# Nine identity products, raw weights in place, a head in pairs, and an early branch in a fused attention and two-layer kernel

## The chip, the cores and the metric

One core of one Trainium2 chip runs the whole program. The metric is the device time of one execution in microseconds (us). The engines are PE (TensorE), PEld (TensorE's weight loads), DVE (VectorE), ACT (ScalarE), POOL (GpSimd) and SP (SyncE, which here issues every DMA). Each engine works through its own instructions in the order written; semaphores order them between engines.

## The reference

Three stages. Attention is a gated recurrence over 768 steps for each of 4 x 8 heads with 48 dimensions; its output is the input of two feed-forward layers of 384 -> 2048 -> 384 over 3072 tokens.

```python
f = 1 / (1 + exp(-f_logit))
for t in range(S):                                  # attention
    state = f[t, :, None] * state + outer(k[t], v[t])
    y[t] = q[t] @ state
h = x @ w_in                                        # layer 1, g is a quadratic spline of h
g = where(h >= 1, h, where(h <= -1, 0, (h + 1)**2 / 4)); x = g @ w_out
h = x @ w2_in                                       # layer 2, g is a rational function of h
g = (a0 + a1*h + a2*h**2 + a3*h**3) / (1 + |b0|*|h| + |b1|*h**2 + 1e-6); out = g @ w2_out
```

## The kernel before

**Attention** is computed in chunks of 128 steps. An *item* is one chunk of one group of 8 heads (4 batches x 2 heads): 6 chunks x 4 groups = 24 items; `chunk_of(i)` names them. For an item ACT turns the gate logits into decay steps (`gate_steps`, L586), DVE multiplies them up (`scan`, L826), ACT and DVE form the inverse (`invert` L599, `newton` L845, `scale_queries` L859), POOL scales the keys (`scale_keys`, L497). PE computes scores (L1031), DVE masks them (L868), PE computes `outputs` (L1047) and transposed keys (`transposes`, L1018), ACT copies these (`copy_keys`, L611), PE forms `deltas` (L1067) and DVE adds them to the `states` (L879). ACT's `round_y` (L619) and DVE's `rest_y` (L893) split y into two fp32r parts, x_hi and x_lo. Part of y is moved between partitions by twelve small DMAs (`move_fourth`, L378).

**The layers** take blocks of 512 tokens, 6 blocks. Every product is three fp32r products: w_hi x_hi, w_hi x_lo and w_lo x_hi. Layer 1 has 16 *tiles* of 128 hidden rows per block, n = 0 to 95: `spline_first(n)` and `spline_second(n)` are nine matmuls of 512 columns each, and ACT and DVE compute the spline between them (`spline_in`, `spline_join`, `spline_hi`, `spline_lo`). Items 4 to 23 are worked into the loop over n, one per window of four tiles: `window_of(n)` gives item 4 + n // 4 and a stage 0 to 3. Stage 0 has the item's transposes and scores, stage 2 its outputs and deltas, stage 3 its rest_y and states. `transposes(i)` for i > 4 wait until item i - 1's states are done. Layer 2 has 8 *units* of 256 hidden rows per block (`rational_first`, `rational_second`, 18 matmuls each, the second four units after the first), and ACT, DVE and POOL steps per unit (`rational_step`).

**Weights** come in 16 pieces per layer (0 to 7 of the first matrix, 8 to 15 of the second; 384 KB each). SP loads a piece into one of two raw buffers, ACT copies it to w_hi rounded (`split_w1`, `split_w2`), POOL subtracts the rest into w_lo in three parts. `ORDER1`, `ORDER2` and `STEPS2` are the orders and steps by hand. Layer 2's pieces take the places of layer 1's: ten are split during layer 1's last block (at steps t in `STEPS2`), six in units 0 to 5 of layer 2's first block. The next block's x is split by ACT and POOL in units 4, 5 and 6 (`split_x2`).

**The head** is what comes ahead of the loop over n: items 0 to 3 and the start of item 4, each engine's order written out (PE from L1181, ACT from L756, DVE from L956, POOL from L560, SP from L408). **The end**: every engine reads a flag that DVE has set in layer 1's last block (growth in range) and jumps over a general program if all is well.

The functions that the change touches, and what calls them:

Of the kernel before, what the change touches and what calls it, by code (L numbers as in the profile page):

```python
# [58 lines left out]
ORDER1 = [m + UNITS * out for m in range(UNITS) for out in range(2)]  # L59
# [9 lines left out]
X2_STEPS = [3, 4, 6]  # L69

# [37 lines left out]
def build(nc, qT, kT, fT, vT, fC, kC, qC, vC, w1, w2, a, b, outT):  # L108
# [3 lines left out]
    with ctx:  # L112
# [9 lines left out]
        w_lo = lay.tile("w_lo", PIECES * WPC, F32R)  # L122
        x_hi = lay.tile("x_hi", [P, KT, 2 * NB], F32R)
# [3 lines left out]
        w_raw = [lay.tile(f"w_raw{u}", WPC) for u in range(2)]  # L127
# [105 lines left out]
        w1_loaded = [sem(f"w1_loaded{r}") for r in range(2)]  # L233
        w1_hi_done = sem("w1_hi_done")
        w1_lo_done = sem("w1_lo_done")
        w2_loaded = [sem(f"w2_loaded{r}") for r in range(2)]
# [94 lines left out]
        def _(sp):  # L331
# [32 lines left out]
            def load_w1(k):  # L364
                if k >= 2:
                    sp.wait_ge(w1_lo_done, SPLITS * (k - 1))
                at = ORDER1[k] * WPC
                sp.dma_start(w_raw[k % 2][:, :], w1[:, at:at + WPC]).then_inc(w1_loaded[k % 2], 16)

            def load_w2(k):  # L370
                if k >= 2:
                    sp.wait_ge(w2_lo_done, SPLITS * (k - 1))
                else:
                    sp.wait_ge(w1_lo_done, SPLITS * PIECES)
                at = ORDER2[k] * WPC
                sp.dma_start(w_raw[k % 2][:, :], w2[:, at:at + WPC]).then_inc(w2_loaded[k % 2], 16)
# [54 lines left out]
            load_f(5)  # L431
            move_fourth(0)
# [4 lines left out]
            load_w1(2)  # L437
            load_q(5)
            load_w1(3)
            load_v(5)  # L440
            load_w1(4)
            sp.dma_start(a_bc[:, :], a.rearrange("(o a) -> o a", o=1).to_broadcast([P, 4])).then_inc(coef_loaded, 16)
            sp.dma_start(b_bc[:, :], b.rearrange("(o a) -> o a", o=1).to_broadcast([P, 2])).then_inc(coef_loaded, 16)
            for n in range(N1):
# [10 lines left out]
                if n + HEAD_PIECES + 2 < PIECES:  # L455
                    load_w1(n + HEAD_PIECES + 2)
                if n % TILES == LAG1 + 1 and n >= TILES:
                    store1(n // TILES - 1)
                t = n - (N1 - TILES)
                if t == 0:  # L460
                    load_x2(0)
                if t in (0, 1):
                    load_w2(t)
                if t in STEPS2:
                    load_w2(STEPS2.index(t) + 2)
            load_x2(1)
            for k in range(len(STEPS2) + 2, PIECES):
                load_w2(k)
# [5 lines left out]
            store2(BLOCKS - 1)  # L474
            sp.wait_ge(flag_set, 1)
            flag = sp.value_load(okflag[0:1, 0:1], min_val=0, max_val=P)
            sp.wait_ge(stored2, 16 * KT * BLOCKS)
            with sp.If(flag < P):
                general.sync_program(sp, qT, kT, fT, vT, xT, x1T, w1, w2, outT)

        @block.gpsimd
        def _(pool):
# [26 lines left out]
            def split_w1(k):  # L509
                pool.wait_ge(w1_hi_done, k + 1)  # L510
                for part in range(SPLITS):
                    own = slice(part * WPC // SPLITS, (part + 1) * WPC // SPLITS)
                    at = slice(ORDER1[k] * WPC + own.start, ORDER1[k] * WPC + own.stop)
                    nc.gpsimd.tensor_tensor(w_lo[:, at], w_raw[k % 2][:, own], w_hi[:, at].bitcast(F32),
                                            ALU.subtract).then_inc(w1_lo_done, 1)

            def split_w2(k):
                m = ORDER2[k]
                pool.wait_ge(w2_hi_done, k + 1)
                if m < UNITS:  # L520
                    pool.wait_ge(h1_ready, N1 - TILES + UW * (m + 1))
                else:
                    pool.wait_ge(multiplied1, N1 - TILES + UW * (m - UNITS + 1))
                for part in range(SPLITS):
                    own = slice(part * WPC // SPLITS, (part + 1) * WPC // SPLITS)
                    at = slice(m * WPC + own.start, m * WPC + own.stop)
                    nc.gpsimd.tensor_tensor(w_lo[:, at], w_raw[k % 2][:, own], w_hi[:, at].bitcast(F32),  # L527
# [37 lines left out]
            split_w1(1)  # L565
            scale_keys(4)
            split_w1(2)
            for n in range(N1):
                i, stage = window_of(n)
                if n + HEAD_PIECES < PIECES:  # L570
                    split_w1(n + HEAD_PIECES)
# [445 lines left out]
        def _(pe):  # L1017
# [179 lines left out]
            for n in range(N1):  # L1197
                i, stage = window_of(n)
                spline_first(n)
                if n == 0:  # L1200
                    deltas(3)
# [298 lines left out]
```

## Time and profile before

| | us |
|---|---|
| median of 3 runs | 930.59 (928.19 to 931.43) |
| the profiled execution | 931.32 |
| its span, first to last instruction | 929.6 |
| PE busy | 894.3 (96%) |
| PEld / DVE / ACT / POOL busy | 737.5 / 666.1 / 632.3 / 277.8 |
| mean granted PE clock | 0.985 of full |

The rows of the profile give a start, a duration, the engine, the source line, and what is written from what, with the number of instructions; the brackets at the end hold the idle time of the engine ahead of the instruction and what ended it. Durations of matmuls overlap: the time from one start to the next is what a matmul costs. An fp32 matmul is recorded as two. A busy PE is not a PE at its peak.

### The profile page before, as it was taken

Reading aid. Unit: us, or ns where it says so; the run is one execution under the profiler, and the core shown is the slowest. Engines: PE = TensorE matmul, PEld = TensorE weight load, DVE = VectorE, ACT = ScalarE, POOL = GpSimd, SP = SyncE. Lnnn points to the kernel's source line nnn. Section 1 sums busy time; section 2 is a strip of 40 time slices with the busy share of each in tenths; the row PEclk is TensorE's granted clock in tenths of the full one; section 3 lists DMA queues with packets and bytes.
Section 4 is the critical chain, followed back from the end, with each engine's and each line's share of the span. In section 5 each row is a group of like instructions: output and inputs, shape, how many; then the busy total and the mean of one; then the engine's idle time right before and its main releaser. Section 6 shows DMA issues by size and latency. Waiting matters only on the chain.

```text
span 929.6 us, 13243 instructions
## 1 busy us (share of the span) xinstructions
PE 894.3 (96%) x4786; PEld 737.5 (79%) x4786; DVE 666.1 (72%) x813; ACT 632.3 (68%) x821; POOL 277.8 (30%) x202
## 2 busy tenths in 40 slices
PE   4799999999999999999999998999999999999996
PEld 3577788888888888888888886888888888888884
DVE  7866656655655566565344799889899889889883
ACT  5566665556555655655577796888787888887881
POOL 3455500000010000000055487235344244353223
PEclk9699999999999999999999998999999999999999
DMA  6434313212211211110233221001001001000001
GB/s 190 117 96 133 103 35 97 58 35 62 59 35 36 85 55 49 58 37 1 69 102 88 83 68 35 1 35 34 0 34 34 23 11 34 34 0 0 34 0 38
DMA packets 27513, 48.72 MB, mean 52 GB/s; under 512 B 5312, under 2 KB 8384, under 8 KB 27456
## 3 DMA queue, kind: packets, MB, share of 16 engines
q1 hardware_dynamic: 27456, 48.00, 17.3%
q8 instruction: 31, 0.51, 0.2%
q14 instruction: 26, 0.21, 0.1%
HBM read 36.18 MB, written 9.44 MB: 49 GB/s over the span
## 4 chain that ended last, share of the span: by engine, by line
PE 79%; DVE 8%; ACT 5%; issue 4%; POOL 3%; POOLq 0%; DMA 0%; SPq 0%; DVEq 0%; ACTq 0%
PE acc L1121 18%; PE acc L1165 18%; PE h_pair L1104 17%; PE at_pair L1143 10%; PE h_pair L1143 10%; PE at_pair L1044 2%; DVE growth L838 2%; PE at_pair L1063 2%; PE at_pair L1058 2%; DVE g L909 1%; POOL g_lo L548 1%; POOL w_lo L527 1%; ACT t L656 1%; ACT t L653 1%; DVE guess L856 1%
## 5 line engine op out<-in xcount | busy, mean ns | idle before, releaser
L548 POOL TENSOR_TENSOR g_lo<-g,g_hi 128x1024 fp32r<-128x1024 f32 x48 | 116.7, 2432 | 222.9 <-DVE t L938 218.4
L909 DVE SCALAR_TENSOR_TENSOR g<-h_pair,t 128x512 f32<-128x512 f32 x96 | 66.4, 691 | 142.1 <-ACT t L656 141.9
L653 ACT ACTIVATE t<-h_pair,half 128x512 f32<-128x512 f32 x96 | 66.0, 688 | 101.1 <-PE h_pair L1104 99.9
L1104 PE MATMUL h_pair<-x_hi,w_hi 128*128 128x512 f32 x288 | 113.6, 394 | 2.8 <-DVE x_lo L902 2.5
L507 POOL TENSOR_TENSOR k_s<-k_in,growth 128x512 f32<-128x512 f32 x22 | 29.0, 1316 | 289.0 <-DVE growth L838 288.2
L1165 PE MATMUL acc<-g_hi,w_hi 128*128 128x512 f32 x288 | 112.5, 390 | 1.9 <-POOL g_lo L548 1.9
L1104 PE MATMUL h_pair<-x_hi,w_lo 128*128 128x512 f32 x288 | 112.9, 392 | 0.0
L1104 PE MATMUL h_pair<-x_lo,w_hi 128*128 128x512 f32 x288 | 112.8, 392 | 0.0
L1165 PE MATMUL acc<-g_lo,w_hi 128*128 128x512 f32 x288 | 112.1, 389 | 0.0
L1165 PE MATMUL acc<-g_hi,w_lo 128*128 128x512 f32 x288 | 112.1, 389 | 0.0
L1121 PE MATMUL acc<-g_hi,w_hi 128*128 128x512 f32 x264 | 107.5, 407 | 0.0
L663 ACT CAST g_hi<-g 128x512 fp32r<-128x512 f32 x88 | 54.6, 621 | 75.3 <-DVE g L909 75.2
L1121 PE MATMUL acc<-g_hi,w_lo 128*128 128x512 f32 x264 | 103.2, 391 | 0.0
L1121 PE MATMUL acc<-g_lo,w_hi 128*128 128x512 f32 x264 | 102.9, 390 | 0.0
L917 DVE TENSOR_TENSOR g_lo<-g,g_hi 128x512 fp32r<-128x512 f32 x88 | 63.0, 716 | 46.7 <-ACT g_hi L663 46.7
L929 DVE SCALAR_TENSOR_TENSOR s<-s,b_abs,g 128x1024 f32<-128x1024 f32 x48 | 66.6, 1388 | 37.8 <-ACT g L709 37.7
L527 POOL TENSOR_TENSOR w_lo<-w_raw,w_hi 128x256 fp32r<-128x256 f32 x48 | 48.1, 1030 | 69.9 <-ACT w_hi L647 66.3
L1104 PEld LDWEIGHTS h_pair<-x_hi,w_hi 128*128 128x128 f32 x288 | 54.5, 189 | 15.4 <-DVE x_lo L902 3.0
L953 DVE SCALAR_TENSOR_TENSOR g<-g,a_bc,t 128x1024 f32<-128x1024 f32 x48 | 65.5, 1364 | 0.0
L1165 PEld LDWEIGHTS acc<-g_hi,w_hi 128*128 128x128 f32 x288 | 54.1, 188 | 14.2 <-POOL g_lo L548 3.1
L1104 PEld LDWEIGHTS h_pair<-x_hi,w_lo 128*128 128x128 f32 x288 | 54.5, 189 | 11.5
L1104 PEld LDWEIGHTS h_pair<-x_lo,w_hi 128*128 128x128 f32 x288 | 54.5, 189 | 11.2
(142 smaller groups left out, 2053.9 us busy)
## 6 DMA issues: line engine op xcount, KB each, us to landing
w_raw<-w SPq DMA_DIRECT2D x32, 384.0 KB, 3.4
f_in<-fC SPq DMA_DIRECT2D x48, 96.0 KB, 2.9
k_in<-kC SPq DMA_DIRECT2D x48, 96.0 KB, 2.4
q_in<-qC SPq DMA_DIRECT2D x48, 96.0 KB, 2.3
mlp_out<-o_sb SPq DMA_DIRECT2D x18, 256.0 KB, 3.3
x_raw<-mlp_out SPq DMA_DIRECT2D x6, 768.0 KB, 4.4
outT<-o_sb SPq DMA_DIRECT2D x18, 256.0 KB, 2.0
v_in<-vC SPq DMA_DIRECT2D x22, 192.0 KB, 2.5
```

What stands on the lines that cost most here:

```text
L527: nc.gpsimd.tensor_tensor(w_lo[:, at], w_raw[k % 2][:, own], w_hi[:, at].bitcast(F32), ALU.subtract).then_inc(w2_lo_done, 1)
L548: nc.gpsimd.tensor_tensor(g2_lo[r][:, :, :], g2[r][:, :, :], g2_hi[r][:, :, :].bitcast(F32), ALU.subtract).then_inc(lo2_ready, 1)
L653: nc.scalar.activation(t1[n % 2][:, :], h1[n % 2], ACT.Relu, scale=0.5, bias=half[:, :]).then_inc(relu1_ready, 1)
L663: nc.scalar.copy(hi, g1[n % 2][:, :]).then_inc(hi1_ready, 1)
L909: nc.vector.scalar_tensor_tensor(out=g1[n % 2][:, :], in0=h1[n % 2], scalar=1.0, in1=t1[n % 2][:, :], op0=ALU.max, op1=ALU.min).then_inc(g ...
L917: nc.vector.tensor_tensor(lo, g1[n % 2][:, :], hi.bitcast(F32), ALU.subtract).then_inc(lo1_ready, 1)
L929: nc.vector.scalar_tensor_tensor(out=s, in0=s, scalar=b_abs[:, 1:2], in1=g, op0=ALU.mult, op1=ALU.add).then_inc(den_ready, 1)
L953: nc.vector.scalar_tensor_tensor(out=g_before, in0=g_before, scalar=a_bc[:, 0:1], in1=t_before, op0=ALU.add, op1=ALU.mult).then_inc(g2_rea ...
L1104: mm = nc.tensor.matmul(h1[n % 2], w[:, at:at + P], x[:, kt, cols], start=(kt == 0 and j == 0), stop=(kt == KT - 1 and j == 2))
L1121: mm = nc.tensor.matmul(acc[o][:, :], w[:, at:at + P], g, start=(t == 0 and j == 0), stop=(t == TILES - 1 and j == 2))
L1143: mm = nc.tensor.matmul(h2[m % 2][:, c * NB:(c + 1) * NB], w[:, at:at + P], x[:, kt, xcols], start=(k == 0), stop=(k == 3 * KT - 1))
L1165: mm = nc.tensor.matmul(acc[o][:, :], w[:, at:at + P], g[m % R2][:, c, :], start=(m == 0 and c == 0 and k == 0), stop=(last and c == UW - ...
```

## The change

It has six parts. (1) `keep_busy`: six fp32 products of the identity with itself ahead of item 2's scores and three ahead of item 3's, into the scores' own PSUM bank, read by nobody and overwritten by the scores. (2) The raw weights lie in w_lo's memory, each piece at its own place with its own semaphore; a load of layer 1 waits for nothing, a load of layer 2 until the old piece has been used. Layer 1's pieces alternate between the matrices. (3) The head is written in pairs: items 2 and 3 together, and the first four tiles and item 4 of the loop unrolled and reordered on ACT, DVE and PE. (4) In the loop, layer 1's pieces are split one tile later. (5) Layer 2's last six pieces go to units 0, 1, 2, 3, 7 and 8 instead of 0 to 5. (6) SP reads the flag ahead of its last store and jumps ahead of the wait for that store; ACT reads it ahead of layer 2.

```diff
-ORDER1 = [m + UNITS * out for m in range(UNITS) for out in range(2)]
+ORDER1 = [0, 1, 8, 2, 9, 3, 10, 4, 11, 5, 12, 6, 13, 7, 14, 15]
+LATE_PIECES = {0: [10], 1: [11], 2: [12], 3: [13], 7: [14], 8: [15]}
         w_lo = lay.tile("w_lo", PIECES * WPC, F32R)
+        lay.at -= 4 * PIECES * WPC
+        w_raw = lay.tile("w_raw", PIECES * WPC)
...
-        w_raw = [lay.tile(f"w_raw{u}", WPC) for u in range(2)]
...
             def load_w1(k):
-                if k >= 2:
-                    sp.wait_ge(w1_lo_done, SPLITS * (k - 1))
-                at = ORDER1[k] * WPC
-                sp.dma_start(w_raw[k % 2][:, :], w1[:, at:at + WPC]).then_inc(w1_loaded[k % 2], 16)
+                at = slice(ORDER1[k] * WPC, (ORDER1[k] + 1) * WPC)
+                sp.dma_start(w_raw[:, at], w1[:, at]).then_inc(w1_loaded[k], 16)
             def load_w2(k):
-                if k >= 2:
-                    sp.wait_ge(w2_lo_done, SPLITS * (k - 1))
+                m = ORDER2[k]
+                if m < UNITS:
+                    sp.wait_ge(h1_ready, LAST_BLOCK + UW * (m + 1))
                 else:
-                    sp.wait_ge(w1_lo_done, SPLITS * PIECES)
+                    sp.wait_ge(multiplied1, LAST_BLOCK + UW * (m - UNITS + 1))
...
+            load_w1(2)
             move_fourth(0)
...
-                if t in (0, 1):
-                    load_w2(t)
-                if t in STEPS2:
-                    load_w2(STEPS2.index(t) + 2)
+                if t + 1 in STEPS2:
+                    load_w2(STEPS2.index(t + 1))
...
-            store2(BLOCKS - 1)
             sp.wait_ge(flag_set, 1)
             flag = sp.value_load(okflag[0:1, 0:1], min_val=0, max_val=P)
+            store2(BLOCKS - 1)
+            with sp.If(flag < P):
+                sp.wait_ge(stored2, 16 * KT * BLOCKS)
+                general.sync_program(sp, qT, kT, fT, vT, xT, x1T, w1, w2, outT)
             sp.wait_ge(stored2, 16 * KT * BLOCKS)
-            with sp.If(flag < P):
-                general.sync_program(sp, qT, kT, fT, vT, xT, x1T, w1, w2, outT)
...  # POOL's and ACT's split_w2 no longer wait for h1_ready or multiplied1
-            late_pieces = range(len(STEPS2), PIECES)
-            for off, piece in enumerate(late_pieces):
-                rational_step(0, off, [piece])
+            for off in range(UNITS + 1):
+                rational_step(0, off, LATE_PIECES.get(off, ()))
...  # ACT, from round_y(0)
-            copy_keys(0) round_y(1) split_w1(0) invert(3) copy_keys(1) round_y(2) copy_keys(2)
-            gate_steps(4) split_w1(1) round_y(3) invert(4) copy_keys(3) split_w1(2) gate_steps(5)
-            for n in range(N1 + LAG1):
+            copy_keys(0) invert(3) round_y(1) copy_keys(1) gate_steps(4) split_w1(0) split_w1(1)
+            round_y(2) round_y(3) copy_keys(2) copy_keys(3) split_w1(2) gate_steps(5)
+            spline_in(0) invert(4) spline_hi(0) spline_in(1) spline_hi(1) copy_keys(4) split_w1(3)
+            spline_in(2) spline_hi(2) invert(5) split_w1(4) spline_in(3) spline_hi(3) round_y(4)
+            gate_steps(6) split_w1(5)
+            for n in range(WINDOW, N1 + LAG1):
...
+            act.wait_ge(flag_set, 1)
             flag = act.value_load(okflag[0:1, 0:1], min_val=0, max_val=P)   # now ahead of layer 2
...  # DVE, from mask(1)
-            rest_y(0) newton(2) scale_queries(2) scan(3) rest_y(1) mask(2) newton(3)
-            scale_queries(3) rest_y(2) mask(3) scan(4) rest_y(3) states(0) newton(4)
-            scale_queries(4) states(1) states(2) states(3)
+            scan(3) rest_y(0) newton(2) scale_queries(2) newton(3) scale_queries(3) mask(2) mask(3)
+            rest_y(1) rest_y(2) rest_y(3) states(0) states(1) scan(4) states(2) states(3)
+            spline_join(0) newton(4) spline_lo(0) scale_queries(4) spline_join(1) mask(4)
+            spline_lo(1) scan(5) spline_join(2) spline_lo(2) newton(5) scale_queries(5)
+            spline_join(3) rest_y(4) states(4) spline_lo(3)
...  # PE
+            def keep_busy(i, count):
+                for _ in range(count):
+                    nc.tensor.matmul(scores_at(i)[0][0][:, 0:P], ident[:, :], ident[:, :], start=True, stop=True)
...  # PE, from transposes(1)
-            scores(2) deltas(0) outputs(2) transposes(2) scores(3) deltas(1) outputs(3)
-            transposes(3) deltas(2)
+            deltas(0) keep_busy(2, 6) scores(2) keep_busy(3, 3) scores(3) outputs(2) outputs(3)
+            transposes(2) transposes(3) deltas(1) deltas(2)
+            spline_first(0) deltas(3) spline_first(1) transposes(4) spline_first(2)
+            spline_second(0) scores(4) spline_first(3) second_half(4) spline_second(1)
```

## Rows read from the trace of the kernel before

**Rows 1.** The page's first part: busy us, share of the span, instructions.
```profile
PE 894.3 (96%) x4786; PEld 737.5 (79%) x4786; DVE 666.1 (72%) x813; ACT 632.3 (68%) x821; POOL 277.8 (30%) x202
```

**Rows 2.** TensorE by stretch: length, busy, granted clock, DMA share, GB/s.
```profile
24.10:26.40 2.30, 0.00 (x0) 1.00 0.18 39
27.00:27.50 0.50, 0.50 (x10) 0.77 0.23 45
...
44.00:44.50 0.50, 0.50 (x5) 0.66 0.46 129
...
574.10:580.00 5.90, 5.90 (x14) 0.50 0.46 133
```

**Rows 3.** The timeline of TensorE in the head.
```profile
38.42 0.79 PE L1104 MATMUL h_pair<-x_hi,w_hi 128*128 128x512 f32 x1 [1.90 <-DVE x_lo L902]
...
49.72 1.05 PE L1058 MATMUL at_pair<-q_s,state 128*128 128x128 f32 x8
50.70 1.08 PE L1063 MATMUL at_pair<-probs,v_in 128*48 128x128 f32 x16
...
58.36 0.39 PE L1104 MATMUL h_pair<-x_hi,w_hi 128*128 128x512 f32 x1
...
62.12 0.63 PE L1028 MATMUL at_bank<-ident,k_s 128*128 128x128 f32 x4 [1.56 <-DVE state L891]
```

**Rows 4.** The chain of waits: start, length, what.
```profile
124.98 2.34 PE h_pair L1104 x9
...
131.13 2.04 PE h_pair L1104 x9
...
642.53 4.08 PE at_pair L1143 x18
```

**Rows 5.** The timeline of TensorE and GpSimd around layer 2's start.
```profile
474.23 2.13 POOL L527 TENSOR_TENSOR w_lo<-w_raw,w_hi 128x256 fp32r<-128x256 f32 x3 [3.53 <-PE h_pair L1104]
...
549.74 2.41 POOL L548 TENSOR_TENSOR g_lo<-g,g_hi 128x1024 fp32r<-128x1024 f32 x1 [1.25 <-DVE t L938]
552.11 5.09 POOL L527 TENSOR_TENSOR w_lo<-w_raw,w_hi 128x256 fp32r<-128x256 f32 x3
...
574.05 0.79 PE L1143 MATMUL at_pair<-x_hi,w_hi 128*128 x1 [3.22 <-POOL x_lo L537]
...
581.15 0.39 PE L1165 MATMUL acc<-g_hi,w_hi 128*128 128x512 f32 x1
...
638.83 2.35 POOL L537 TENSOR_TENSOR x_lo<-x_raw,x_hi 128x512 f32 x1
```

**Rows 6.** The end: last stores, then single instructions by line (ns, start us).
```profile
920.69 3.05 SPq L406 DMA_DIRECT2D outT<-o_sb  x3
...
L478 SPq COMPARE_BRANCH  x1: 50/50/50, 926.6 to 926.6; - x1
...
L112 ACTq DRAIN  x1: 80/80/80, 926.8 to 926.8; - x1
L112 SPq DRAIN  x1: 48/48/48, 929.3 to 929.3; - x1
...
L810 ACTq TENSOR_LOAD <-okflag x1: 743/743/743, 922.8 to 922.8; - x1
```

**Rows 7.** The timeline of VectorE in the head.
```profile
22.20 1.36 DVE L838 TENSOR_TENSOR_SCAN growth<-growth,zero 128x128 f32<-128x128 f32 x4
...
33.94 2.58 DVE L838 TENSOR_TENSOR_SCAN growth<-growth,ends,zero 128x128 f32<-128x128 f32 x4 [1.27 <-ACT growth L597]
...
36.97 1.40 DVE L902 TENSOR_TENSOR x_lo<-at_bank,x_hi 48x512 fp32r<-48x512 f32 x2
```

**Rows 8.** ScalarE in layer 1's last block; layer 2's loads from issue to landing.
```profile
481.50 0.68 ACT L653 ACTIVATE t<-h_pair,half 128x512 f32<-128x512 f32 x1
...
486.77 0.83 ACT L647 CAST w_hi<-w_raw 128x768 fp32r<-128x768 f32 x1
...
DMA to landing us min/median/max: 2.9/3.3/5.4
```

More of the change, by code:

```diff
@@ L511, in split_w1 @@
                 for part in range(SPLITS):
-                    own = slice(part * WPC // SPLITS, (part + 1) * WPC // SPLITS)
-                    at = slice(ORDER1[k] * WPC + own.start, ORDER1[k] * WPC + own.stop)
-                    nc.gpsimd.tensor_tensor(w_lo[:, at], w_raw[k % 2][:, own], w_hi[:, at].bitcast(F32),
+                    at = slice(ORDER1[k] * WPC + part * WPC // SPLITS, ORDER1[k] * WPC + (part + 1) * WPC // SPLITS)
+                    nc.gpsimd.tensor_tensor(w_lo[:, at], w_raw[:, at], w_hi[:, at].bitcast(F32),
                                             ALU.subtract).then_inc(w1_lo_done, 1)
@@ L964, in _ @@
             mask(1)
+            scan(3)
             rest_y(0)
@@ L967, in _ @@
             scale_queries(2)
[L968 to L970 removed]
             newton(3)
             scale_queries(3)
+            mask(2)
+            mask(3)
+            rest_y(1)
             rest_y(2)
[L974 to L975 removed]
             rest_y(3)
             states(0)
[L978 to L979 removed]
             states(1)
+            scan(4)
             states(2)
             states(3)
[L983 removed]
+            spline_join(0)
+            newton(4)
+            spline_lo(0)
+            scale_queries(4)
+            spline_join(1)
+            mask(4)
+            spline_lo(1)
+            scan(5)
+            spline_join(2)
+            spline_lo(2)
+            newton(5)
+            scale_queries(5)
+            spline_join(3)
+            rest_y(4)
+            states(4)
+            spline_lo(3)
+            for n in range(WINDOW, N1):
                 i, stage = window_of(n)
@@ L1186, in _ @@
             transposes(1)
+            deltas(0)
+            keep_busy(2, 6)
             scores(2)
-            deltas(0)
+            keep_busy(3, 3)
+            scores(3)
             outputs(2)
+            outputs(3)
             transposes(2)
-            scores(3)
+            transposes(3)
             deltas(1)
-            outputs(3)
-            transposes(3)
             deltas(2)
-            due = 0
-            for n in range(N1):
+            spline_first(0)
+            deltas(3)
+            spline_first(1)
+            transposes(4)
+            spline_first(2)
+            spline_second(0)
+            scores(4)
+            spline_first(3)
+            second_half(4)
+            spline_second(1)
+            due = LAG1
+            for n in range(WINDOW, N1):
                 i, stage = window_of(n)
                 spline_first(n)
-                if n == 0:
-                    deltas(3)
                 if stage == 0:
@@ L1205, in _ @@
                     second_half(i)
-                if n >= LAG1 and n not in HOLD:
+                if n not in HOLD:
                     spline_second(due)
```

97 lines of the change are left out of this document (47 added, 50 removed).

## The prediction

> **What bounds the kernel now.** I read the shares first, then the granted clock by stretch, then each engine's instructions at the three places where TensorE is not busy. [rows 1] give TensorE 894.3 of 929.6 us busy, so only its gaps and its low clock can be won. [rows 2] show the two low stretches. TensorE did nothing from 24.10 to 26.40; the granted clock then fell at 27.0 to 27.5 from 1.00 to 0.50, which is 1.2 instead of 2.4 GHz, and came back at 44.0 to 44.5. It also worked at 0.50 from 574.1 to 580, behind a second gap. [rows 3] follow the head: first product of spline tile 0 at 38.42, released by VectorE; tile 4 at 58.36; the transposes of item 5 at 62.12 after 1.56 us of waiting for the state sums. From 124.98 (tile 16) on, groups of nine products follow each other every 2.04 us and the rational units of four such groups every 8.16 [rows 4]: there TensorE is the bound. The second gap is the wait of 3.22 us in [rows 5] for GpSimd's x_lo, because GpSimd had 5.09 us of weight split, 2.35 of x_lo and 2.41 of g_lo, 9.85 in a unit of 8.16. The third loss is the end in [rows 6]: a branch at 926.6, the drain at 929.3.
>
> **The head.** Added: nine fp32 identity products. The nearest row of that shape (128x128 weights, 128 columns) is the state product in [rows 3]: 8 records, two per product, in 0.98 us from its start to its follower's at 50.70, so 0.245 us each, 1.47 for six and 0.74 for three. Other bound: they cost nothing where TensorE waits anyway. The rest is order. I walk the new one with durations of [rows 3, 7] and of the same groups of the head at the full clock.
>
> Until 18.9 us nothing changes. VectorE then does scan 3 (1.36), the rest of y 0 (0.61), and two items' inverses and queries (2.05 each): queries 2 are ready at 23.0, queries 3 at 25.1. TensorE has item 1's transposes done at 21.8, item 0's deltas (0.47) at 22.3, six products until 23.8, scores 2 (1.09) until 24.9, three products until 25.6, scores 3 until 26.7. Masks 2 and 3 (1.20 each) end at 26.3 and 27.95, outputs 2 at 27.8 and 3 at 29.1, transposes at 30.2. Three times 1.42 for the rests of y 1 to 3 end at 32.2; the moved rows of x, issued as before, are there by then. So spline tile 0 starts at 32.3, 6.1 earlier, and at the full clock: TensorE's longest gap since 19.9 is under 1 us, where the old one was 2.4. The nine products lie in the wait for the queries except 0.6 us, which VectorE's masks inherit and which is in the walk.
>
> Then tile 0 until 34.3, deltas 3, tile 1 until 36.8. Scan 4 (up to 2.58 beside GpSimd) ends at 36.0, its keys (1.28) at 37.3, transposes 4 at 37.9, tile 2 at 40.4, second product 0 at 42.4, scores 4 at 43.5, tile 3, outputs and deltas 4 (2.36) at 47.9, second product 1 at 50.0, tile 4 at 52.1. The old tile 4 ended at 60.4. This is 8.3 us ahead, but the vector side isn't: mask 4 must wait for scores 4 (43.6 to 44.8), then come lo 1, scan 5 (until 47.4), join 2 (48.0), ScalarE's hi 2, inverse 5 (1.29), weight split (0.74) and tile 3 (1.3) until 52.0, join 3, hi 3, rounding of y 4 (0.50), rest of y 4 and state sums 4 until 56.3. TensorE's transposes of item 5 wait for these sums: from 52.1 to 56.3, 4.2 us instead of 1.56. Queued behind this wait are scores 5 and all spline products; ScalarE and VectorE wait for them. **Gain at this point: 62.12 - 56.3 = 5.8 us.** Carried on with the same durations to tile 16, it is 6.8 (118.2 against 124.98), since the next two waits for state sums shrink to 0 and 0.7. The same arithmetic in the old order gives tile 4 at 58.1 and tile 16 at 124.7, where the rows have 58.36 and 124.98. With no slowing of VectorE beside GpSimd it gives a gain of 5.2; the bounds are 5.2 and 6.8, and I take 6.8, as the rows do show that slowing (scan 2.58 against 1.36).
>
> This holds if the clock stays up. Gaps of 2.4 and 3.2 us were each followed by 0.50 [rows 2], so I expect it to fall in this 4.2 us gap, and to come back some 6 us after work resumes, as it did after 574.05. At half rate transposes, scores and a spline group take 1.04 + 1.7 + 3.84 instead of 0.56 + 1.09 + 2.04, 2.9 us; if a second group is caught, 4.7. Of the 6.8 remain 3.9 or 2.1. **I take 3.5.**
>
> By the Trainium skill, TensorE: Matmul & The Clock Gate (Part 1, the section on what is actually happening), the number of matmuls before the clock is released varies between runs of one kernel. The trace agrees as far as one execution can: 7.0, 5.7 and 6.1 us of work preceded the three rises. By that rule the 3.9 and the 2.1 can both occur in runs of the same kernel.
>
> **The first weights.** Raw pieces now land in w_lo's own place, so no load waits for a split, and the pieces' order alternates. ScalarE casts 13 pieces in the windows as before (three of them in the unrolled part), one tile later each; each first-matrix piece is ready three tiles before its use, each second-matrix piece about two. What hides this is that distance. Taken 0; bounds 0 and +0.8 (one cast of 0.83, as in [rows 8], on the path once).
>
> **The second weights in place.** The load of a piece now waits until the old piece is no longer read, and two raw buffers no longer run ahead. The tightest is piece 3: tile 87's product is there at 481.50 at the latest, the cast starts at 486.77, 5.3 us later; loads land in 3.3 us, at most 5.4 [rows 8]. Taken 0; bounds 0 and 0.2 us for each of seven such pieces, 1.4. SP's queue behind these waits holds only the next pieces, load_x2 and the last stores, none of them due within 8 us. ScalarE's earlier read of the flag costs 0.74 + 0.17 + 0.02 (the first of them in [rows 6]) at 509.9, where it delays unit 0; TensorE uses the result four units later (32 us), so 0.
>
> **The late pieces.** Pieces 14 and 15 move from units 4 and 5 to units 7 and 8. GpSimd in units 4 to 6 then has 2.41 + 2.35 = 4.8 us, as in every later block, and in 7 and 8 2.41 + 5.09 = 7.5, both under 8.16. In a later block the third x_lo ends at 641.2, 1.3 us ahead of its matmul at 642.5 [rows 4, 5]. Here pieces 12 and 13 have already put item 2's g_lo 1.4 us late (549.74), and VectorE, the cause, has 0.7 us idle per later unit to win it back: the third x_lo ends between 569.8 and 570.8, its matmul is due at 570.67. So the gap goes but for 0.2 at most, too short for the clock: the group behind it starts at 570.67 + 4.08 = 574.75 instead of 581.15 [rows 5]. **Gain 6.4 us**: 3.4 of gap with its restart, 3.0 of low clock. Next late would be the second products of units 6 and 7, which need pieces 14 and 15 at 591 and 599; the splits end near 572 and 580. Lower bound 3.2, if a shorter wait stays.
>
> By the Trainium skill, GPSIMD Engine Reference (1, Specifications), GpSimd's SBUF interface is shared with VectorE and contended by vector instructions with two SBUF inputs. This speaks against putting the pieces into units 7 and 8, where VectorE is 90% busy. The trace agrees: three splits took 5.09 there and 2.13 elsewhere [rows 5]. Taken at 2.13, units 4 and 5 would never have been late; at 5.09 the new place still fits.
>
> **The end.** SP's flag read moves ahead of the last store and the branch ahead of the wait for it. Before: last issue done at 923.74, wait for landing until 926.6, branch, 2.6 us to the drain [rows 6]. After: branch at 923.8, 2.6 us, landing at 926.6 meanwhile, end near 926.9 instead of 929.6. ScalarE's branch comes 1.0 earlier (drain near 925.9). Gain 2.6; the jump may be slower beside the store's traffic, down to 1.5. **I take 2.5.**
>
> **Sum.** 3.5 + 6.4 + 2.5 = 12.4. The profiled execution took 931.32, 1.7 more than its span; it stands 0.7 above the median 930.59 and inside 928.19 to 931.43. 931.32 - 12.4 = 918.9; half of the 0.7 off for the median: **918.5 us**.
>
> **Rivals.**
> 1. The clock survives the gap at 52 us. For: TensorE is dense on both sides; against: both old gaps, which were shorter. Head 6.8, sum 15.7, 915.6 us.
> 2. The nine products don't hold the clock at 27 us. For: they are small, and some waits stay around them; against: TensorE is over 85% busy from 19.9 on. Then the clock is low from 27 to 44 as before; the same walk puts tile 16 at 125.3, 0.5 later than the old order: sum 8.4, 922.9 us.
> 3. The gap at 571 stays, since the third x_lo has only 1.3 us of slack in the steady state and starts here 1.4 late. For: these two numbers; against: what units 4 and 5 no longer do. Sum 6.0, 925.3 us; a gap of 1 us without a fall of the clock leaves 5.4 of the 6.4.
> 4. Slower: layer 2's loads. Once they can't start before the old piece is free, ScalarE, which casts between two tiles, stops for each of seven pieces, and TensorE with it. Slack is 1.9 us over the usual 3.3; it decides from 5.3, and costs all of the 12.4 at 7.1 us per load (seven times 1.8). At 7.8 us per load, 918.5 + 7 x 2.5 = 936 us. Against: the longest of 16 was 5.4.
>
> **How the numbers follow.** Forecast 0.55, rival 1 0.20, rival 2 0.12, rival 3 0.06, rival 4 0.03, something unseen 0.04. Range: the forecast's own is 916.5 to 921; I reach to rival 1 with all terms at their best, 913.5, and past rival 2 to 924.5. A measurement of this kernel tells about 0.3%, 2.8 us, from no change. Faster takes the forecast, rivals 1, 2 and nearly all of 3: 0.93; the same 0.04; slower 0.03.
>
> **What would show it.** Head: granted clock 1.00 from 27 to 44, tile 0 near 32.3, transposes 5 near 56.3 after a wait of about 4 us, 0.50 behind it, tile 16 near 121. Transition: no gap and no 0.50 between 505 and the last unit, the third x_lo of block 1 done before 570.7. End: last landing to the drain under 0.5 us. Wrong would be: 0.50 at 27 to 44; ScalarE waiting for w_raw loads; a wait for x_lo at unit 8; a start of tile 16 later than 124.98.

## The result, and the profile after

| | us |
|---|---|
| changed kernel, median of 4 runs | 919.29 (918.73 to 920.17) |
| kernel before, median of 4 runs | 930.88 (928.19 to 931.43) |
| ratio | 0.9882 [0.9860, 0.9904] |
| profiled execution / its span | 920.17 / 918.4 |

The kernel became 1.2% faster, 11.6 us by the medians. The numbers in brackets behind a ratio are its 95% interval. The changed kernel's four runs form two pairs: 918.73 twice, at a mean granted clock of 0.997, and 919.84 and 920.17 at 0.995; the profiled one is the slowest. The two profiled spans, 929.6 and 918.4, differ by 11.2: 3.0 us in the head, 5.6 at layer 2's start, 2.6 at the end. The forecast of 918.5 had 3.5, 6.4 and 2.5, 12.4 in all.

The page of the changed kernel, first part, against [rows 1]:

```profile
PE 890.6 (97%) x4804; PEld 734.9 (80%) x4804; DVE 663.7 (72%) x813; ACT 632.3 (69%) x821; POOL 276.9 (30%) x202
```

TensorE has 18 more records (nine fp32 products of two each) and is nevertheless busy for 3.7 us less, since less of its work runs at the low clock. The windows on TensorE, against [rows 2] (length, busy, granted clock, DMA share, GB/s):

```profile
27.00:44.00 17.00, 15.16 (x144) 1.00 0.61 176
...
53.00:57.00 4.00, 0.53 (x4) 0.96 0.17 62
57.00:64.00 7.00, 7.00 (x31) 0.53 0.23 52
...
115.00:123.00 8.00, 6.05 (x27) 1.00 0.33 93
...
560.00:582.00 22.00, 21.45 (x95) 1.00 0.12 36
```

The stretch from 27 to 44, which was at 0.50, is at 1.00. One low stretch is left in the head, behind the gap at 53; the one in layer 2 has gone. The timeline of TensorE, against [rows 3]:

```profile
21.61 1.60 PE L1103 MATMUL acc<-ident 128*128 128x128 f32 x12
23.76 1.16 PE L1066 MATMUL acc<-q_s,o_sb 48*128 48x128 f32 x16 [0.54 <-DVE q_s L873]
24.85 0.94 PE L1103 MATMUL at_bank<-ident 128*128 128x128 f32 x6
...
32.62 0.50 PE L1131 MATMUL h_pair<-x_hi,w_hi 128*128 128x512 f32 x1 [0.34 <-DVE x_lo L910]
...
56.56 0.78 PE L1050 MATMUL at_bank<-ident,k_s 128*128 128x128 f32 x3 [3.47 <-DVE state L899]
```

Spline tile 0 starts at 32.62 instead of 38.42; item 5's transposes at 56.56 instead of 62.12. Tile 16, in the chain of waits against [rows 4], starts at 121.95 instead of 124.98. The chain gives what released it:

```profile
118.44 0.69 DVE q_s L862
...
119.15 0.70 DVE guess L864
...
120.49 0.68 DVE x_lo L910
...
121.20 0.70 DVE x_lo L910
...
121.95 2.34 PE h_pair L1131 x9
```

VectorE sets this point, with the next item's query steps (q_s, guess) ahead of the x_lo that tile 16 needs; TensorE waits 1.95 us for it. At layer 2's start the timelines of GpSimd, VectorE and TensorE, against [rows 5], read:

```profile
549.04 2.29 POOL L535 TENSOR_TENSOR x_lo<-x_raw,x_hi 128x512 fp32r<-128x512 f32 x1
...
565.67 2.27 POOL L535 TENSOR_TENSOR x_lo<-x_raw,x_hi 128x512 fp32r<-128x512 f32 x1
...
573.96 5.09 POOL L525 TENSOR_TENSOR w_lo<-w_raw,w_hi 128x256 fp32r<-128x256 f32 x3
...
550.10 2.31 DVE L937 SCALAR_TENSOR_TENSOR s<-s,b_abs,g 128x1024 f32<-128x1024 f32 x1
...
592.40 1.28 DVE L937 SCALAR_TENSOR_TENSOR s<-s,b_abs,g 128x1024 f32<-128x1024 f32 x1
...
568.34 0.49 PE L1170 MATMUL at_pair<-x_hi,w_hi 128*128 x1 [0.55 <-POOL x_lo L535]
```

The wait for x_lo is 0.55 us where it was 3.22. The end in the timeline, against [rows 6]:

```profile
912.07 3.05 SPq L409 DMA_DIRECT2D outT<-o_sb  x3
...
913.74 0.39 PE L1192 MATMUL acc<-g_hi,w_lo 128*128 128x512 f32 x1
914.16 0.60 ACT L682 ACTIVATE o_sb<-acc 128x512 f32<-128x512 f32 x1 [0.76 <-PE acc L1192]
```

And the branch, among the single instructions by line (ns, start us):

```profile
L479 SPq COMPARE_BRANCH  x1: 50/50/50, 915.2 to 915.2; - x1
```

SyncE now branches at 915.2, as soon as its last store is issued (912.07 + 3.05), and no longer waits for it to land first. From the end of TensorE's last product to the end of the span it is 918.4 - 914.13 = 4.3 us; before it was 6.8 (929.6 - 922.75).

### The profile page after: what moved, and what is told of

The parts are those of the page before. It is cut to its first block, busy times and chain, and to the rows that moved or that the text cites. A ratio compares the mean times of both kernels' runs of the same rounds, so it can differ in the third digit from the quotient of the medians.

```text
span 918.4 us, 13245 instructions
## 1 busy us (share of the span) xinstructions
PE 890.6 (97%) x4804; PEld 734.9 (80%) x4804; DVE 663.7 (72%) x813; ACT 632.3 (69%) x821; POOL 276.9 (30%) x202
## 4 chain that ended last, share of the span: by engine, by line
PE 81%; DVE 9%; ACT 4%; issue 4%; POOL 1%; POOLq 0%; DMA 0%; DVEq 0%; SPq 0%; ACTq 0%
PE acc L1148 19%; PE acc L1192 18%; PE h_pair L1131 17%; PE at_pair L1170 10%; PE h_pair L1170 10%; PE at_pair L1066 2%; PE at_pair L1085 2%; DVE growth L846 2%; PE at_pair L1080 2%; DVE g L917 1%; POOL g_lo L546 1%; ACT t L649 1%; ACT t L646 1%; PE at_bank L1050 1%; DVE probs L885 1%
## 5 line engine op out<-in xcount | busy, mean ns | idle before, releaser
L937 DVE SCALAR_TENSOR_TENSOR s<-s,b_abs,g 128x1024 f32<-128x1024 f32 x48 | 69.4, 1446 | 31.8 <-ACT g L702 31.7
L961 DVE SCALAR_TENSOR_TENSOR g<-g,a_bc,t 128x1024 f32<-128x1024 f32 x48 | 63.6, 1326 | 0.0
L1192 PEld LDWEIGHTS acc<-g_hi,w_lo 128*128 128x128 f32 x288 | 54.0, 188 | 11.2
```

The costliest lines, as they stand in the source:

```text
L937: nc.vector.scalar_tensor_tensor(out=s, in0=s, scalar=b_abs[:, 1:2], in1=g, op0=ALU.mult, op1=ALU.add).then_inc(den_ready, 1)
L961: nc.vector.scalar_tensor_tensor(out=g_before, in0=g_before, scalar=a_bc[:, 0:1], in1=t_before, op0=ALU.add, op1=ALU.mult).then_inc(g2_rea ...
L1192: mm = nc.tensor.matmul(acc[o][:, :], w[:, at:at + P], g[m % R2][:, c, :], start=(m == 0 and c == 0 and k == 0), stop=(last and c == UW - ...
```

## The experiments

Each was timed in turn with the kernel before on the same chip, and the ratios compare the two; medians of different chips are not compared directly. "By ratio" below means the ratio, or the difference of two ratios, times 930 us.

| run | median us (runs) | before us | ratio |
|---|---|---|---|
| e1_no_products | 920.57 (4) | 929.89 | 0.9891 [0.9874, 0.9907] |
| e2_products_old_order | 930.01 (12) | 929.89 | 0.9997 [0.9982, 1.0013] |
| e3_fill_gap | 918.83 (4) | 929.89 | 0.9877 [0.9862, 0.9892] |
| e4_sums_early | 918.40 (4) | 929.89 | 0.9874 [0.9859, 0.9889] |
| e5_late_alone | 924.88 (5) | 931.30 | 0.9929 [0.9915, 0.9943] |
| e7_pieces_earlier | 917.98 (4) | 931.30 | 0.9871 [0.9853, 0.9889] |
| e9_fill_both | 917.19 (4) | 931.30 | 0.9853 [0.9838, 0.9868] |
| e10_sums_fill_pieces | 915.98 (5) | 931.30 | 0.9839 [0.9826, 0.9853] |
| e6_end_alone | 927.72 (12) | 929.31 | 0.9981 [0.9969, 0.9993] |
| e11_in_place_alone | 930.06 (12) | 929.31 | 1.0013 [1.0001, 1.0025] |
| e12_best_no_products | 916.45 (4) | 929.31 | 0.9862 [0.9847, 0.9876] |
| e13_head_only | 925.22 (8) | 929.95 | 0.9957 [0.9942, 0.9972] |

**What are the nine products worth?** Two runs: the changed kernel without them, and the kernel before with them.

```diff
-            keep_busy(2, 6)
-            keep_busy(3, 3)      # e1; e2 adds both ahead of scores(2) and scores(3) in the old order
```

> The changed kernel without its nine identity products; all else is kept. Theory A (the products hold TensorE's clock in the head): the granted clock falls to 0.50 somewhere between 24 and 30 us and comes back near 44; tile 0 and what follows run at half rate until then, tile 16 starts near 125 instead of 121.95, and the time is 923 to 924 us. Rival B (the order in pairs alone is dense enough, the products only fill a wait): the clock stays at 1.00, tile 16 starts within 0.5 of 121.95, the time is 919 us.

> The kernel before with the nine identity products at the same two places (six ahead of item 2's scores, three ahead of item 3's); order, weights and the rest as before. Theory A (products and order are both needed): the gap behind item 0's deltas is only cut from 2.4 to some 1.5 us, the clock falls near 27 as before, and the time stays at 930 to 932 us. Rival B (products alone hold the clock): 1.00 at 30 us, tile 4 starts near 53.5 instead of 58.36, but the vector side gives most of it back in a longer wait at item 5's transposes (3.6 us, and a fall of the clock there): 928 to 930 us.

The windows on TensorE without the products (e1):

```profile
26.00:27.00 1.00, 1.00 (x18) 0.96 0.19 37
27.00:30.00 3.00, 3.00 (x31) 0.50 0.24 54
30.00:32.00 2.00, 2.00 (x30) 0.92 0.58 173
```

The clock does fall without them, at 26.9 where it fell at 27.3 before, but it is back after 3.4 us and not after 17. Tile 16 starts at 122.95 instead of 121.95: 1.0 us. By the ratios the products are worth 0.8 us, and that difference alone is not told apart from nothing. Theory A's fall came, its 923 to 924 us didn't. In the old order (e2):

```profile
27.00:30.00 3.00, 3.00 (x20) 0.50 0.24 53
30.00:32.00 2.00, 1.96 (x34) 0.93 0.63 185
...
36.00:40.00 4.00, 1.70 (x4) 0.64 0.53 151
40.00:44.00 4.00, 4.00 (x26) 0.51 0.16 28
```

Here the low stretch of 17 us is two shorter ones, the second behind the wait of 3.2 us for x_lo ahead of tile 0, and the time is unchanged (tile 16 at 124.83; before 124.98). The products need not have done that: e6 below has the old head without them, and its profile too has two stretches (10.2 and 3.4 us). TensorE is at 1.00 from 30.3 to 37.1 in e2, and tile 0 still starts at 38.30 (before 38.42), released by VectorE's x_lo: up to tile 0 the old head waited for VectorE, and its low clock there was hidden. So it is the order that brings tile 0 from 38.4 to 33.3 us in e1 and ends the stretch from 27 to 44; the products take at most a short stretch away.

**What does the gap at 53 us cost?** e3 fills it with thirteen more such products; e4 shortens it, by putting item 4's rounding and state sums ahead of item 5's inverse on ScalarE and VectorE.

```diff
+                if n == WINDOW:
+                    fill(13)                # e3: ident x ident into at_pair, ahead of transposes(5)
...
-            newton(5) scale_queries(5) spline_join(3) rest_y(4) states(4) spline_lo(3)    # e4, DVE
+            rest_y(4) states(4) newton(5) scale_queries(5) spline_join(3) spline_lo(3)
-            invert(5) split_w1(4) spline_in(3) spline_hi(3) round_y(4)                    # e4, ACT
+            round_y(4) invert(5) spline_in(3) split_w1(4) spline_hi(3)
```

> The changed kernel with 13 more unread identity products (0.248 us each, 3.2 us) in the 3.47 us in which TensorE waits for item 4's state sums ahead of item 5's transposes. Nothing is made ready earlier. Theory A (what this gap costs is the clock behind it): granted clock 1.00 from 56 to 64 us, tile 16 near 118.5 instead of 121.95, time 915.5 to 916.5 us. Rival B (the cost is the wait itself, since ScalarE and VectorE set the pace here): clock at 1.00, but tile 16 within 1 us of 121.95 and the time above 918 us.

> The changed kernel with the wait itself taken away: VectorE does the rest of y and the state sums of item 4 ahead of item 5's inverse, ScalarE rounds y of item 4 ahead of its inverse 5, and the weight split follows tile 3's first step. Theory A (the wait costs nothing, only the clock behind it; ScalarE and VectorE then set the pace up to tile 16): transposes 5 start at 53.1 with no wait, the clock stays at 1.00, later waits of 1 to 2 us come at items 6 and 7, tile 16 near 118, time 915.5 to 916.5 us, the same as when the gap is filled. Rival B (the wait is worth its 3.5 us too): tile 16 near 115, time 912 to 913 us.

The filled kernel (e3) in the timeline of TensorE:

```profile
52.96 3.06 PE L1108 MATMUL at_pair<-ident 128*128 128x128 f32 x26
56.63 0.63 PE L1050 MATMUL at_bank<-ident,k_s 128*128 128x128 f32 x4 [0.61 <-DVE state L899]
```

in its windows:

```profile
57.00:64.00 7.00, 7.00 (x44) 1.00 0.23 52
...
119.00:122.50 3.50, 3.50 (x9) 0.51 0.08 25
```

and in its chain of waits:

```profile
118.85 3.91 PE h_pair L1136 x9
```

The chain of the reordered one (e4):

```profile
118.46 2.35 PE h_pair L1131 x9
```

and its window:

```profile
119.00:122.50 3.50, 3.50 (x29) 1.00 0.00 1
```

The transposes start no earlier in e3 (56.63), only the clock is kept, and tile 16 comes 3.1 us earlier, at 118.85. In these two profiles that is the whole of the 2.9 us that I had put on the low clock. e4, which shortens the waits for state sums from 3.6 to 2.1 us in all and keeps the clock, gets tile 16 to 118.46, only 0.4 earlier than e3: VectorE sets the pace up to there. But neither run is 3 us faster than the changed kernel; by ratio they gain 0.5 to 0.7, and the 915.5 to 916.5 us of both theories A were missed. Two things account for that. The first is in the changed kernel itself: the profile of e7, a kernel with the same head (its edit is in layer 2), has the low stretch behind the same gap, but of 3.4 us, where the changed kernel's lasted 6.8:

```profile
57.00:64.00 7.00, 7.00 (x37) 0.76 0.24 53
...
120.31 0.50 PE L1131 MATMUL h_pair<-x_hi,w_hi 128*128 128x512 f32 x1 [2.00 <-DVE x_lo L910]
```

Its tile 16 starts at 120.31, so keeping the clock here is worth 1.5 us in some executions and 3.1 in others; the changed kernel's two pairs of runs, 1.1 to 1.4 us apart, would fit that, though only one of the four has a trace. The second: in e3's profile the 2.0 us of waiting ahead of tile 16 was followed by 0.50, and its nine products took 3.91 us instead of 2.34. In e4's profile (916.67 us) the same gap was followed by 1.00; its three other runs took 918.2 to 918.6 at a lower mean clock (0.997 to 0.998 against 0.999), which would fit the fall, but they left no trace. By the Trainium skill, TensorE: Matmul & The Clock Gate (Part 1, the section on what is actually happening), the point of release varies between runs of one kernel. The trace agrees: behind one gap of one head the clock came back after 3.4 us in e7's profile and after 6.8 in the changed kernel's. The fall varies here too: the gap ahead of tile 16 lost the clock in e3's profile and kept it in e4's.

**Both gaps filled.** e9 is e3 with seven products more, ahead of tile 16.

```diff
+                if n == TILES:
+                    fill(7)
```

> The changed kernel with fp32 identity products written as the others: thirteen ahead of item 5's transposes (the gap at 53 us) and seven ahead of tile 16's first product (the 2.0 us gap at 117 us that was followed by clock 0.50 when only the first gap was filled). Theory A (each low stretch behind a gap costs about half its length; the gap itself costs nothing because VectorE sets the pace): granted clock 1.00 from 20 us to beyond tile 16, tile 16's group 2.0 to 2.4 us long, time 916.9 (918.83 less 1.9), in all 2.3 to 2.8 under the changed kernel's 919.3. Theory B (the products push the work behind them and what the clock gives is taken back by VectorE or GpSimd later): 918.5 to 919.3, with tile 16's group at 2.3 and a longer wait elsewhere before 130 us. Seven products cost 1.7 us where the gap is shorter than that, so up to 0.3 later if the gap is 1.5.

The timeline of TensorE:

```profile
116.65 1.72 PE L1108 MATMUL at_pair<-ident 128*128 128x128 f32 x14
118.81 0.50 PE L1136 MATMUL h_pair<-x_hi,w_hi 128*128 128x512 f32 x1 [0.43 <-DVE x_lo L910]
```

and the window around it:

```profile
115.00:123.00 8.00, 7.57 (x53) 1.00 0.18 49
```

Theory A holds: tile 16 at 118.81, clock 1.000 in all four runs, which lie within 0.4 us of each other. By ratio it is 2.2 us faster than e3, and 2.7 faster than the changed kernel.

**The transition.** e5 moves the late pieces in the kernel before and nothing else. e7 moves pieces 11, 12 and 13 of the changed kernel one unit earlier.

```diff
-            late_pieces = range(len(STEPS2), PIECES)                                     # e5
+LATE_PIECES = {0: [10], 1: [11], 2: [12], 3: [13], 7: [14], 8: [15]}
...
-LATE_PIECES = {0: [10], 1: [11], 2: [12], 3: [13], 7: [14], 8: [15]}                     # e7
+LATE_PIECES = {0: [10, 11], 1: [12], 2: [13], 7: [14], 8: [15]}
```

> The kernel before with nothing changed but the units of layer 2's last six pieces: 0, 1, 2, 3, 7 and 8 instead of 0 to 5. Theory A (the gap at 571 us comes from pieces 14 and 15 in units 4 and 5, and the change took 5.6 us there): 5.6 less than before, 924.3 against 929.9, and no stretch at granted clock 0.50 in layer 2; with all 6.4 us of my step, 923.5. Rival (part of the gap went because raw weights lie in place and GpSimd no longer waits for the old piece's products): 3 to 4.5 less, 925.5 to 927, and a wait over 1 us for x_lo at unit 8.

> The changed kernel with layer 2's late pieces 10 and 11 both in unit 0, 12 in unit 1, 13 in unit 2, 14 and 15 in units 7 and 8 as in it. Theory A (the 0.6 us wait for x_lo at unit 8 is GpSimd's lag behind, brought on by piece 13 in unit 3, and VectorE has no time left to win it back): the wait is 0.1 or less and the time 0.6 to 0.8 under the changed kernel's, 918.5 to 918.7. Theory B (GpSimd starts each g_lo when VectorE has t ready, so its place comes from VectorE's own pace and not from the pieces): the wait stays at 0.5 to 0.6, 919.2 to 919.4. Bad case: two pieces in unit 0 make TensorE wait there for second products 0 by 1 to 3 us.

The first product of unit 8, which waits for x_lo, in the timeline of e5:

```profile
571.24 0.49 PE L1142 MATMUL at_pair<-x_hi,w_hi 128*128 x1 [0.54 <-POOL x_lo L538]
```

and of e7, where no wait is left:

```profile
566.01 0.39 PE L1170 MATMUL at_pair<-x_hi,w_hi 128*128 x1
```

e5 gained 6.6 us [5.3, 7.9] by ratio (6.4 by medians), and has the wait of 0.54 of the changed kernel: the rival that laid part of this on the raw weights falls, since they aren't in place here. e7's profile has no wait and tells theory A right; its time is 1.0 us below the changed kernel by ratio, and that alone is inside the interval. Its profiled 917.71 us can't be set against the changed kernel's 920.17 for these pieces, since 1.6 us of that is the shorter low stretch in the head shown above.

**The end alone** (e6), and **the raw weights alone** (e11).

```diff
-            store2(BLOCKS - 1)                                                           # e6, SP
             sp.wait_ge(flag_set, 1)
             flag = sp.value_load(okflag[0:1, 0:1], min_val=0, max_val=P)
-            sp.wait_ge(stored2, 16 * KT * BLOCKS)
+            store2(BLOCKS - 1)
             with sp.If(flag < P):
+                sp.wait_ge(stored2, 16 * KT * BLOCKS)
...
+        lay.at -= 4 * PIECES * WPC                                                       # e11
+        w_raw = lay.tile("w_raw", PIECES * WPC)
-                if k >= 2:
-                    sp.wait_ge(w1_lo_done, SPLITS * (k - 1))
```

> The kernel before with SyncE's flag read ahead of its last store and its branch ahead of the wait for that store, and ScalarE's flag read ahead of layer 2. Theory A (SyncE's taken branch of 2.6 us goes beside the landing of the store): last TensorE product to the end of the span 4.2 to 4.3 us instead of 6.84, time 2.5 less than before. Rival (the branch becomes slower beside the store's traffic, or ScalarE's own branch ends last): 1 to 1.9 less, with ScalarE's drain as the last record.

> The kernel before with its raw weights in w_lo's place and nothing else of the change: a load of layer 1 waits for nothing, one of layer 2 for the last product of the old piece, and neither ScalarE nor GpSimd waits for those products again. Theory A (my step: nothing): within 0.8 us of before. Rival 1 (my slower case: ScalarE stands for the loads that now start later): 1.4 to 17 more, with waits of ScalarE for w_raw in layer 1's last block. Rival 2 (it helps: loads in the head start earlier and the first splits with them): 1 to 2 less.

In e6's profile the last product ends at 919.63 and the span at 923.9: 4.3 us, as theory A has it. Its median came out 1.8 us below before by ratio, [0.7, 2.9], which doesn't contradict 2.6 but doesn't show it either. The reason why twelve runs don't settle 2.6 us is in the same profile, at layer 2's start, first in the timeline:

```profile
573.61 0.49 PE L1146 MATMUL at_pair<-x_hi,w_hi 128*128 x1 [3.21 <-POOL x_lo L539]
```

then in the window behind it:

```profile
574.00:580.00 6.00, 6.00 (x28) 1.00 0.42 131
```

The gap of 3.2 us is there, and the clock stays at 1.00 behind it, where [rows 2] have 0.50 for 5.9 us. So the 3.0 us of low clock in this place are paid in some executions and not in others (in e11's and e13's profiles the stretch there is 3.4 us long instead of 6.8), and runs of the kernel before lie between 926.4 and 932.1 at mean clocks of 0.994 to 0.983. e11 is 1.2 us slower than before by ratio, [0.1, 2.3]. Its waits are those of before: TensorE's tile 16 at 124.93, 3.2 us for x_lo, no wait of ScalarE for w_raw in layer 1's last block. My slower case doesn't show, and neither does a gain; what the 1.2 would be, if it is more than scatter, stays open.

**The head, with the raw weights in place.** e13 undoes the late pieces and SyncE's early branch.

```diff
-LATE_PIECES = {0: [10], 1: [11], 2: [12], 3: [13], 7: [14], 8: [15]}
+LATE_PIECES = {0: [10], 1: [11], 2: [12], 3: [13], 4: [14], 5: [15]}
...
+            sp.wait_ge(stored2, 16 * KT * BLOCKS)
             with sp.If(flag < P):
-                sp.wait_ge(stored2, 16 * KT * BLOCKS)
```

> The changed kernel with layer 2's late pieces back in units 0 to 5 and SyncE's branch back behind the wait for the last store: what is left is the head with its nine products and the raw weights in place. Theory A (the head is worth 3.0, as tile 16's start says): 3.0 less than before, 926 to 927.5 against 929.5 to 931, tile 16 within 0.5 of 121.95, and the wait of 3.2 us for x_lo at unit 8 back. With my prediction's term: 3.5 less. Rival (the head's gain in single runs is mostly VectorE's waits moved, and the terms of the parts don't add): 1 less or nothing. The clock behind the wait for x_lo may fall or not, as it did in one profile and not in another, which makes the runs spread by 3 us.

The chain of its profiled execution, the slowest of eight at 928.84:

```profile
122.03 3.92 PE h_pair L1131 x9
```

and its timeline at layer 2's start:

```profile
572.62 0.79 PE L1170 MATMUL at_pair<-x_hi,w_hi 128*128 x1 [3.19 <-POOL x_lo L535]
```

It lost the clock three times, behind the gaps at 53, at 120 and at 569. Five of the eight runs lie at 925.0 to 925.4 with a mean clock of 0.995. By ratio the head is worth 4.0 us [2.6, 5.4], which holds the 3.0 of the two traces, my 3.5, and the 4.7 that e7's profile of the same head gives (124.98 - 120.31).

**A faster kernel.** e10 puts together e4's order, the seven products ahead of tile 16 and e7's pieces; e12 is the same without the nine products.

> Meant as the best version: the changed kernel with item 4's state sums ahead of item 5's inverse on VectorE and its rounding ahead of item 5's inverse on ScalarE (918.40 alone), seven identity products ahead of tile 16, and layer 2's pieces 10 and 11 in unit 0, 12 in unit 1, 13 in unit 2. If the terms add: 918.4 less 1.4 (the clock no longer falls at 117 us, in four runs of five) less 0.6 (the wait for x_lo at unit 8) = 916.4, range 915.5 to 917.2. Rival: the terms overlap with VectorE's pace and it stays at 917.5 or more, with the same waits moved.

> The fastest kernel so far (sums of item 4 early, seven identity products ahead of tile 16, layer 2's pieces in units 0, 0, 1, 2, 7, 8; 915.98) without the nine products ahead of items 2 and 3's scores. Theory A (they are worth only the short low clock at 27 to 30 us, and that is on the path): 1.0 to 1.3 more, 917.0 to 917.3, with 0.50 from 27 to 30.2. Theory B (here the spline tiles behind have slack, so that low stretch is hidden): 915.9 to 916.3. Against both, my prediction's rival 2: 7 more.

e10 is the fastest kernel of this study: 915.98, 1.6% under before and, by ratio, 4.0 us under the changed kernel; its five runs lie between 915.78 and 916.39 at clocks of 0.999 to 1.000. e12's windows in its profiled execution, at 918.07:

```profile
27.00:30.00 3.00, 3.00 (x32) 0.50 0.25 55
30.00:32.00 2.00, 2.00 (x17) 0.50 0.61 166
```

Its four runs spread over 2.2 us (915.89 to 918.07, clocks 1.000 to 0.996): two of them are as fast as e10's, so the clock can stay up without the products too. The profiled one has the low clock for 6.8 us (25.6 to 32.4), where e1, with the same order of work on TensorE up to there, had 3.4, and its tile 16 starts at 120.59 against 118.89 in e10: 1.7 us. The products make the fast case the regular one, if four runs against five may be read so; by ratio e12 is 2.1 us behind e10, and the intervals still touch.

## Why the prediction was right, step by step

**The head, tile 0 and the transposes.** The walk gave 32.3 and 56.3, the trace 32.62 and 56.56, with 3.5 us of waiting instead of 4.2. The price of 0.245 us per fp32 product held: in e2, where the scores follow without a wait, six took 1.43 us from 21.43 to 22.86, 0.24 each. The clock fell behind the gap at 53 and stayed low for 6.8 us (56.7 to 63.5); e3 shows 3.1 us for it against my 2.9. In e7's profile it is 3.4 us and 1.5, less than the smaller of my two cases. My reading of the work ahead of the three old rises, 7.0, 5.7 and 6.1 us, was a little short: to the rises themselves it is 7.6, 5.9 and 6.2.

**The head, tile 16.** Predicted near 121, measured 121.95; the gain is 3.0, not 3.5 (4.7 in e7's profile, 4.0 by e13's ratio). The step that was too good is "the next two waits for state sums shrink to 0 and 0.7". Those waits did shrink, to 0.17 in all, but a wait of 1.95 for x_lo came behind them that the walk didn't have as a place of risk. The 6.8 that I gave for a clock that stays up was nearly there in e3 (124.98 - 118.85 = 6.1).

**Rival 1 had the mechanism right and the time wrong.** With the first gap's clock kept I gave 915.6. e3 did just that and came to 918.83, because the next gap, ahead of tile 16, takes 1.6 us back in the same way, and the late pieces gave less: 6.1 - 1.6 + 5.6 + 2.6 = 12.7, and 931.3 - 12.7 = 918.6. e9 shows the rest of it.

**Rival 2 was mis-sized, and with it the worth of the products.** I wrote that without them "the clock is low from 27 to 44 as before" and put 922.9 on it. e1 shows the fall and no such length: 3.4 us, and 6.8 in e12's profile. I had taken the 17 us of one execution of the old order over to the new one. Only the old order shows 17 (before, e5, e11; e6 has 10.2), which speaks for its waits keeping the clock low, but equal code had lengths that differ by a factor of two, so what sets the length isn't shown. The argument "TensorE is over 85% busy from 19.9 on" was right for the changed kernel (6.43 of 7.00 us) and mattered little to its gain. The title of the change puts the products first; the runs put them last.

**The late pieces.** 6.4 predicted, 5.6 between the two traces, 6.6 [5.3, 7.9] in e5. The step that failed is "VectorE has 0.7 us idle per later unit to win it back". That idle time isn't free while x_lo is split. I had read it in rows like these of the kernel before, DVE first, then GpSimd:

```profile
640.70 1.56 DVE L929 SCALAR_TENSOR_TENSOR s<-s,b_abs,g 128x1024 f32<-128x1024 f32 x1 [0.67 <-ACT g L709]
...
636.46 2.42 POOL L548 TENSOR_TENSOR g_lo<-g,g_hi 128x1024 fp32r<-128x1024 f32 x1 [3.56 <-DVE t L938]
...
644.74 2.41 POOL L548 TENSOR_TENSOR g_lo<-g,g_hi 128x1024 fp32r<-128x1024 f32 x1 [3.56 <-DVE t L938]
```

With [rows 5], x_lo ended at 641.18 and the s step that began during it at 642.26, 1.08 us later. In the changed kernel the s steps of units 4 to 6 end 1.08 or 1.09 us after x_lo too, and so they do in e7. Where VectorE has no idle time ahead of s, s begins earlier within x_lo and just takes longer: 2.31 us instead of 1.56, and 1.28 where GpSimd is idle. Behind s comes t, t releases GpSimd's g_lo, and the next x_lo comes behind g_lo. One such round takes 8.3 us: g_lo starts at 546.67, 554.98 and 563.28 here, every 8.30 us in e7, and 8.28 apart in the rows above. That is more than the 8.16 of a unit, so no lag can shrink in these units. The result is the wait of 0.55 us that I had limited to 0.2. I had named such a wait as a sign of being wrong, and it appeared. e7 removed it by starting without the lag. The 3.0 of the low clock here I had taken as certain; e6 shows it isn't, so this term is 6.4 or 3.4 in single runs. A smaller slip: I had the splits of pieces 14 and 15 end near 572 and 580, 19 us ahead of their use; they end at 579.05 and 587.75, and the products that need them start at 588.86 and 597.02, so 9 us were left.

**The end.** 2.5 predicted, 2.6 in the traces of the changed kernel and of e6.

**Raw weights in place** were put at 0, and no wait of the traces speaks against it; **rival 4** (slower through layer 2's loads) didn't occur: ScalarE waits for no w_raw in layer 1's last block. **Rival 3** (the gap stays) fell, though the small number on which it rested, the 1.4 us of lag, was real.

**How much of the hit is luck.** The terms for the head and for layer 2's start were 0.5 and 0.8 us too high against the two profiles, both in the same direction; set against the profiled execution the forecast was 918.9 and the measurement 920.17. What brought the median within 0.8 us of 918.5 is the 0.35 us taken off for it and the two runs at 918.73, in which the clock was low for less time. The mechanisms were right but for the lag at layer 2's start and the length of the low stretch without the products; a hit within 1 us is closer than single low stretches of varying length let one promise.

## What to carry to other kernels

A gap costs its own length only where nothing behind it has slack; what it may cost beside that is the clock, and neither whether it falls nor how long it stays low is fixed by the kernel, so one trace of it is a sample. Read both apart: fill the gap with products that nobody reads, and if its follower starts no earlier but later stages do, it was the clock. After closing one gap look for the next of similar length, since it takes over, and judge by the mean clock of each run as well as by the median. When you count on an engine to win back lag, follow the whole round of releases between it and its neighbour and compare the length of the round with that of a unit; idle time in which it could not have started anything sooner doesn't count.

## What was not expected of the hardware

- The same gap loses the clock in one execution and not in another: 3.2 us at 570 (0.50 behind it in the kernel before, 1.00 in e6), 2.0 us ahead of tile 16 (0.51 in e3, lost in e13 too, 1.00 in e4 and in the changed kernel).
- Low stretches lasted 3.4, 6.8, 10.2 and 17.1 us, and equal code had different ones: behind the gap at 53 us 6.8 in the changed kernel, e1 and e13 and 3.4 in e7; near 26 us 3.4 in e1 and 6.8 in e12; in the old order 17.1 before, in e5 and in e11, and 10.2 in e6.
- A vector instruction of 128x1024 took 1.42 to 2.31 us beside GpSimd's x_lo split and 1.28 alone; however early it started, it ended 1.08 or 1.09 us after the split. The split itself took 1.30 us at 476 us in the kernel before and 2.3 in layer 2. GpSimd's three weight parts took 5.09 beside the vector steps in units 7 and 8 and 2.13 at 474 us in layer 1's last block.
- Keeping the clock makes a kernel steady: the runs of e9 span 0.4 us, those of the kernel before nearly 6.
